# Second gated layer of tiles 0 and 1 with held weights and 512 moving tokens, turned back by VectorE during the next tile

## The chip, the cores and the metric

The program runs on one core of a Trainium2 chip. A core has a matrix engine (TensorE, PE in the profile, with PEld for its weight loads), a vector engine (VectorE, DVE), a scalar engine (ScalarE, ACT), GpSimd (POOL) and a queue engine (SyncE, SP) that issues nearly all DMAs here. Each engine runs its own instructions in order; between engines the order is kept by semaphores. SBUF holds 128 partitions of working memory, PSUM holds what PE writes. The metric is the device time of the whole program in microseconds (us), lower being better.

## The reference

Attention with a decay, then a feed-forward layer with a squared ReLU, then a gated feed-forward layer with an RMS norm in front of it, all in float32:

```python
# 4 batches, 8 heads, 768 tokens, 64 wide; afterwards 3072 tokens of 512 features
state = gamma * state + outer(k[t], v[t]);  y[t] = scale * q[t] @ state
h = maximum(x @ w_in, 0);  x = h * h @ w_out                 # 512 -> 2048 -> 512
rms = sqrt(mean(x * x, axis=-1) + 1e-6);  xn = x / rms * rms_g
g = xn @ w_gate;  silu = g * sigmoid(g);  val = xn @ w_val   # 512 -> 1536, twice
out = silu * val @ w_out                                     # 1536 -> 512
```

## The kernel before, in words

Each float32 matrix product is made of seven products of half the size (a Strassen scheme with 7 instead of 8: `OPERAND`, `ITEMS`), and each operand is split into a high and a low float32r part, so that every small product is three matmuls (`three`, L785 to L789). PSUM holds the accumulators X, Y, Z (two banks of 512 columns each); the seven products k = 0 to 6 go to X, Z, Y, X, Y, Z, Y in that order.

The 3072 tokens are three tiles of 1024 tokens, and a tile has two halves, n = 0 and 1, of 512 tokens. After the attention come two layers, each for t = 0, 1, 2. A layer has front runs and then one back run.

- A **front run** (`front_run` on every engine) is seven products of 12 matmuls with 512 moving columns. The second layer (`front2_run` on DVE) has six front runs q = 0 to 5 a tile. When product 0 is done, ACT copies X into Y (`seed`, L982). Product 2 accumulates into Y and so waits for `seeded`, while `seed` waits for `y_taken` of the run before: DVE's last read of Y in that run (`tail`, L1484 to L1491). Between lie ACT's silu (L1014) and a cast of weights (`high_w`, L915). DVE also adds up four weight sums for the next run (`sum_w`, L1361 to L1369).
- A **back run** (`back_run`) multiplies the hidden layer, which lies feature by token in `hid`, with the output weights. It has 21 groups in the second layer (7 products of G2 = 3 groups) and 28 in the first. For each group ACT casts a high part of a hidden operand (`high_hop`, L975), DVE makes the low part (`low_hop`, L1315) in one of three places, DVE also combines operands for later groups (`combine_hop`), and SP fetches a prepared weight item of 512 KB (`load_items`, L474) into one of four places.

In the back run of the first layer the weights are held in PE (stationary) and 512 tokens move: 12 matmuls of 512 columns a group, and the result lies feature by token. In the second layer it is the other way round (L850 to L855): 128 tokens are held and the 256 columns of the weights move, 24 matmuls a group, and the result lies token by feature as `out` needs it. There the norm's factor `rinv` is one number per partition and is applied while X, Y, Z are read: ACT's `scale_tokens` (L986, four instructions of 256 columns) and DVE's L1608 and L1621. A result (A, Dd, Bb, C are the four quarters: two halves of the tokens by two halves of the features) goes to `out_sb`, which is `hid[:, 6:8]`, and SP stores it with `store_out` within the same back run, the last quarter early in the next tile.

The order on each engine is the order of the code. In a front run SP first waits for the last weight part of the run (`w_lo`), issues the next 1 MB of raw weights (`load_raw_w`, L402), then other loads; in run q = 5 of tiles 0 and 1 it also loads 2 MB for the next tile's front (`load_front`, L510), and then the first four items of the back run.

Of the kernel before, what the change touches and what calls it, by code (L numbers as in the profile page):

```python
# [1 line left out]

# [7 lines left out]
ALU = mybir.AluOpType  # L10
# [109 lines left out]
def build(nc, qkv, decay_mask, decay_q, decay_s, decay_k, w_f1, w_f2, w_b, rms_g, out):  # L120
# [6 lines left out]
    with ExitStack() as ctx:  # L127
# [18 lines left out]
        warm = sb("warm", [P, 1])  # L146
        rinv_t = sb("rinv_t", [P, TILES, 8])
        sums_q = sb("sums_q", [P, 32])
# [49 lines left out]
        z_taken = sem("z_taken")  # L198
        seeded = sem("seeded")
        p5_saved = sem("p5_saved")  # L200
        u2_saved = sem("u2_saved")
# [153 lines left out]
        def stored_chunks():  # L355
            return [(b, c) for b in range(B) for c in range(CH) if not (b < 2 and c < 4)]

        def tokens(ps):
# [29 lines left out]
        def _(sp):  # L388
# [134 lines left out]
            def store_out(t, i):  # L523

                s = (A, Dd, Bb, C)[i]
                m, n = divmod(s, 2)
                if s == A:
                    sp.wait_ge(x_taken, run_b2(t) + 1)
                elif s == C and t == TILES - 1:
                    for tb in range(4):  # L530
                        row = CH * (n + 2 * (tb // 2)) + 4 + tb % 2
                        sp.wait_ge(last_scaled, tb + 1)
                        sp.dma_start(out_v[:, row, m, :], out_sb[:, s, tb, :]).then_inc(out_stored, 16)
                    return
                elif s == C:
                    sp.wait_ge(y_taken, run_b2(t) + 1)
# [4 lines left out]
                if t < 2:  # L541
                    row = CH * (2 * t + n)
                    sp.dma_start(out_v[:, row:row + 4, m, :], out_sb[:, s]).then_inc(out_stored, 16)
                    return
# [11 lines left out]
            def spread_rinv(t):  # L556

                sp.wait_ge(rinv_turned, t + 1)
                by_block = rinv_dram[t].rearrange("(k s i) -> s k i", s=4, i=32)
                for i in range(4):  # L560
                    sp.dma_start(by_block[i], rinv_q[8 * i:8 * i + 8, :]).then_inc(rinv_stored[t], 16)
                for i in range(4):
                    sp.dma_start(rinv_t[32 * i:32 * i + 32, t, :], rinv_r[:, i, :]).then_inc(rinv_t_loaded[t], 16)

# [10 lines left out]
            def front_run(m, bk=None):  # L575
# [51 lines left out]
            for t in range(TILES):  # L627
                bk = BackRun(t, True)
                for q in range(R2):
                    front_run(M1 + R2 * t + q, bk if q == R2 - 1 else None)  # L630
                load_items(bk, 0, 8)
                if t + 1 < TILES:
                    load_rinv_b(t + 1)
                load_items(bk, 8, 17)
                store_out(t, 0)
                load_items(bk, 17, 20)
                store_out(t, 1)
                load_items(bk, 20, 21)
                store_out(t, 2)
            store_out(TILES - 1, 3)  # L640
            sp.wait_ge(out_stored, 16 * (4 * (TILES - 1) + 10))

# [69 lines left out]
        def _(pe):  # L712
# [111 lines left out]
            def back_run(bk):  # L824

                for n in range(bk.groups):
# [46 lines left out]
        def _(act):  # L873
# [109 lines left out]

            def scale_tokens(dst, ps, t, n):
                for tb in range(4):
                    op = nc.scalar.activation(dst[:, tb, :], tokens(ps)[:, tb, :], ACT.Copy,  # L986
                                              scale=rinv_t[:, t, 4 * n + tb:4 * n + tb + 1])
                return op

            def save_p5(run, scaled=None):  # L990
# [3 lines left out]
                if scaled is None:  # L994
                    nc.scalar.copy(p5[:], Z[:]).then_inc(p5_saved, 1)
                else:
                    scale_tokens(tokens(p5), Z, scaled, 1).then_inc(p5_saved, 1)

            def save_u2(run, scaled=None):
# [4 lines left out]
                if scaled is None:  # L1004
                    nc.scalar.copy(u2[:], Y[:]).then_inc(u2_saved, 1)
                else:
                    scale_tokens(tokens(u2), Y, scaled, 1).then_inc(u2_saved, 1)

# [13 lines left out]
            def tail(run):  # L1022
# [19 lines left out]
                elif t == TILES - 1:  # L1042
                    for tb in range(4):
                        if tb % 2 == 0:
                            act.wait_ge(last_done, tb // 2 + 1)
                        nc.scalar.activation(out_sb[:, C, tb, :], tokens(Y)[:, tb, :], ACT.Copy,
                                             scale=rinv_t[:, t, tb:tb + 1]).then_inc(last_scaled, 1)
# [76 lines left out]
            def back_run(bk):  # L1124

                t, ng, run = bk.t, bk.ng, bk.run
                for n in range(bk.groups):
# [10 lines left out]
                    if not bk.second and t and n == 19:  # L1138
                        root(t - 1)
                    if n == 2 * ng and bk.second:  # L1140
                        act.wait_ge(rinv_t_loaded[t], 64)
                    if n == 2 * ng:
                        save_p5(run, t if bk.second else None)
                    if n == 3 * ng:
                        save_u2(run, t if bk.second else None)
                    if bk.next_front < 2 * TILES:
# [3 lines left out]
                    if n == 4 * ng:  # L1150
                        act.wait_ge(*done(run, 3))
                        if bk.second:
# [3 lines left out]
                            else:  # L1156
                                act.wait_ge(out_stored, 64 * t)
                            scale_tokens(out_sb[:, A], X, t, 0).then_inc(x_taken, 1)
                        else:
# [49 lines left out]
        def _(dve):  # L1209
# [326 lines left out]
            def front2_run(run, m, t, q, bk):  # L1536
# [38 lines left out]
                if t == 0 and q == 1:  # L1575
                    mean_square(TILES - 1)
                if bk:
                    low_hop(bk, 1)

            def back_run(bk):  # L1580

                t, ng, run = bk.t, bk.ng, bk.run
                for n in range(bk.groups):
# [13 lines left out]
                    if n == 5 * ng:  # L1597
                        dve.wait_ge(*done(run, 4))
                        dve.wait_ge(p5_saved, run + 1)
                        if bk.second:  # L1600
                            dve.wait_ge(rinv_t_loaded[t], 64)
                            if t == 0:
                                for j in range(4):
                                    dve.wait_ge(kept[j], 16 * len(range(j, 28, 4)))
                            else:
                                dve.wait_ge(out_stored, 64 * t)
                            for tb in range(4):
                                op = nc.vector.scalar_tensor_tensor(  # L1608
                                    out_sb[:, Dd, tb, :], tokens(Y)[:, tb, :], rinv_t[:, t, 4 + tb:5 + tb],
                                    tokens(p5)[:, tb, :], ALU.mult, ALU.add)  # L1610
                            op.then_inc(c22_done, 1)
# [4 lines left out]
                    if n == 6 * ng:  # L1616
                        dve.wait_ge(*done(run, 5))
                        dve.wait_ge(u2_saved, run + 1)
                        if bk.second:
                            for tb in range(4):  # L1620
                                op = nc.vector.scalar_tensor_tensor(  # L1621
                                    out_sb[:, Bb, tb, :], tokens(Z)[:, tb, :], rinv_t[:, t, 4 + tb:5 + tb],
                                    tokens(u2)[:, tb, :], ALU.mult, ALU.add)
                            op.then_inc(z_taken, 1)
# [90 lines left out]
```

## Time and profile before

| | before |
|---|---|
| time, median of 3 runs | 1083.81 us (1083.79 to 1085.39) |
| profiled execution | 1083.72 us |
| its span, first to last instruction | 1081.9 us |
| PE busy | 1071.8 us (99%) |
| DVE busy | 870.9 us (80%) |
| ACT busy | 606.0 us (56%) |
| POOL busy | 335.2 us (31%) |
| granted TensorE clock | 1.000 of full speed |

The span is taken inside the profiled execution, which lasts 1.82 us longer than it. "Busy" of PE counts overlapping matmuls with modelled ends, so how fast matmuls really follow each other is read from their start times. In a row of a timeline the first number is the start in us, the second the duration; "idle before" is time the engine had nothing to do, with what ended it. Starts of successive instructions on DVE lie closer than their durations, since an instruction's end overlaps the next one's begin.

### The profile page before, as it was taken

How to read it: one execution, taken by the hardware profiler on the slowest of the kernel's cores; microseconds unless marked ns; L12 is line 12 of the kernel's file. 1: busy time of each engine (PE TensorE's matmuls, PEld its weight loads, DVE VectorE, ACT ScalarE, POOL GpSimd, SP SyncE). 2: the span in 40 equal slices, each digit the busy share in tenths (PEclk: the TensorE clock that was granted, in tenths of full speed). 3: DMA queues.
4: the chain of work that ended last, by engine and by line, in shares of the span. 5: the costliest groups of instructions: out<-in, count | busy, mean ns of one | idle time of the engine just before them, and what ended most of it. 6: DMA issues, size and time to landing. Idle time of an engine off the chain costs nothing.

```text
span 1081.9 us, 16730 instructions
## 1 busy us (share of the span) xinstructions
PE 1071.8 (99%) x6492; PEld 920.7 (85%) x6492; DVE 870.9 (80%) x926; ACT 606.0 (56%) x926; POOL 335.2 (31%) x240
## 2 busy tenths in 40 slices
PE   8999999999999999999999999999999999999998
PEld 7888788888888888888888888998888998888898
DVE  4686999878979879889899988878675976867684
ACT  5886565466644666554664545646454555544453
POOL 1764552004450005430034653005444002544000
PEclk9999999999999999999999999999999999999999
DMA  9999548763447644465642336553114563120355
GB/s 355 381 405 410 214 180 284 235 215 117 175 156 238 216 150 163 149 236 197 224 148 92 122 113 234 195 176 99 39 62 161 199 204 116 40 77 1 117 185 185
DMA packets 68301, 196.49 MB, mean 182 GB/s; under 512 B 7680, under 2 KB 22016, under 8 KB 63360
## 3 DMA queue, kind: packets, MB, share of 16 engines
q1 hardware_dynamic: 65776, 191.22, 50.2%
q10 hardware_dynamic: 2448, 4.22, 1.0%
q8 instruction: 52, 0.85, 0.3%
q14 instruction: 25, 0.20, 0.1%
HBM read 152.87 MB, written 42.48 MB: 181 GB/s over the span
## 4 chain that ended last, share of the span: by engine, by line
PE 92%; DMA 3%; ACT 2%; DVE 1%; issue 1%; POOL 1%; ACTq 0%; SPq 0%; DVEq 0%; POOLq 0%
PE Y L787 13%; PE Y L788 13%; PE Y L789 13%; PE Z L787 8%; PE X L787 8%; PE X L788 8%; PE X L789 8%; PE Z L788 8%; PE Z L789 8%; DMA item_scratch<-ops 2%; PE Z L746 1%; PE Z L736 1%; ACT k_dec L903 1%; PE R L763 1%; DMA kv_sb<-qkv 1%
## 5 line engine op out<-in xcount | busy, mean ns | idle before, releaser
L648 POOL TENSOR_TENSOR w_ops<-raw_w,w_ops 128x512 fp32r<-128x512 f32 x90 | 127.6, 1418 | 500.6 <-ACT w_ops L915 500.5
L975 ACT CAST ops<-hid 128x1024 fp32r<-128x1024 f32 x147 | 154.1, 1048 | 162.6 <-PE Z L789 55.8
L1315 DVE TENSOR_TENSOR ops<-hid,ops 128x1024 fp32r<-128x1024 f32 x147 | 179.5, 1221 | 50.1 <-ACT ops L975 49.4
L648 POOL TENSOR_TENSOR w_ops<-sums_w,w_ops 128x512 fp32r<-128x512 f32 x120 | 172.8, 1442 | 128.5 <-ACT w_ops L915 128.0
L787 PE MATMUL Y<-ops,w_ops 128*128 128x512 f32 x360 | 140.3, 390 | 1.6 <-DVE hid L1511 1.6
L789 PE MATMUL Y<-ops,w_ops 128*128 128x512 f32 x360 | 140.1, 389 | 0.0
L788 PE MATMUL Y<-ops,w_ops 128*128 128x512 f32 x360 | 140.1, 389 | 0.0
L787 PE MATMUL Y<-ops 128*128 128x256 f32 (+1 forms) x360 | 117.1, 325 | 0.0
L788 PE MATMUL Y<-ops 128*128 128x256 f32 (+1 forms) x360 | 117.1, 325 | 0.0
L789 PE MATMUL Y<-ops 128*128 128x256 f32 (+1 forms) x360 | 117.1, 325 | 0.0
L1014 ACT ACTIVATE gt<-gt 128x512 f32<-128x512 f32 x72 | 45.1, 633 | 118.4 <-DVE gt L1574 41.0
L915 ACT CAST w_ops<-sums_w 128x512 fp32r<-128x512 f32 x120 | 74.3, 621 | 45.2 <-PE Y L789 17.3
L787 PE MATMUL X<-ops,w_ops 128*128 128x512 f32 x240 | 93.4, 389 | 0.0
L788 PE MATMUL X<-ops,w_ops 128*128 128x512 f32 x240 | 93.4, 389 | 0.0
L789 PE MATMUL Z<-ops,w_ops 128*128 128x512 f32 x240 | 93.4, 389 | 0.0
L787 PE MATMUL Z<-ops,w_ops 128*128 128x512 f32 x240 | 93.4, 389 | 0.0
L788 PE MATMUL Z<-ops,w_ops 128*128 128x512 f32 x240 | 93.4, 389 | 0.0
L789 PE MATMUL X<-ops,w_ops 128*128 128x512 f32 x240 | 93.4, 389 | 0.0
L787 PEld LDWEIGHTS Y<-ops,w_ops 128*128 128x128 f32 x360 | 67.6, 188 | 16.5 <-DVE hid L1511 2.3
L1240 DVE TENSOR_TENSOR ops<-raw,ops 128x1024 fp32r<-128x1024 f32 x39 | 56.2, 1446 | 30.8 <-ACT ops L934 30.6
L789 PEld LDWEIGHTS Y<-ops,w_ops 128*128 128x128 f32 x360 | 67.6, 188 | 14.2
L788 PEld LDWEIGHTS Y<-ops,w_ops 128*128 128x128 f32 x360 | 67.6, 188 | 13.8
(159 smaller groups left out, 2475.4 us busy)
## 6 DMA issues: line engine op xcount, KB each, us to landing
ops<-item_scratch SPq DMA_DIRECT2D x147, 512.0 KB, 4.0
raw_w<-w_f SPq DMA_DIRECT2D x30, 1024.0 KB, 4.9
item_scratch<-hid SPq DMA_DIRECT2D x30, 512.0 KB, 3.1
qk_sb<-qkv SPq DMA_DIRECT2D x24, 512.0 KB, 8.5
kv_sb<-qkv SPq DMA_DIRECT2D x20, 512.0 KB, 8.6
y_scratch<-hid SPq DMA_DIRECT2D x12, 512.0 KB, 5.8
raw<-y_scratch SPq DMA_DIRECT2D x3, 2048.0 KB, 9.1
raw<-w_b SPq DMA_DIRECT2D x5, 1024.0 KB, 5.0
```

Of the source, the lines that this page charges most:

```text
L648: nc.gpsimd.tensor_tensor(w_ops[:, k, 1], front_w_source(m, k), f32(w_ops[:, k, 0]), ALU.subtract).then_inc(w_lo, 1)
L736: nc.tensor.matmul(y_ps[rows, p * P:(p + 1) * P], state[rows, p, :], q_dec[rows, c % 2, p * P:(p + 1) * P], start=(p == 0), stop=False, sk ...
L746: mm = nc.tensor.matmul(y_ps[rows, cols], kv_sb[:, n % KVR, V, h * D:(h + 1) * D], masked[:, c % 2, h % 2, cols], start=(c == 0 and h < 2) ...
L763: mm = nc.tensor.matmul(state_ps[head_rows(h), D * p:D * p + D], k_dec[:, c % 2, cols], kv_sb[:, n % KVR, V, cols], start=(c == 0 and p == ...
L787: nc.tensor.matmul(dst, left_hi, right_hi, start=start, stop=False, skip_group_check=True)
L788: nc.tensor.matmul(dst, left_hi, right_lo, start=False, stop=False, skip_group_check=True)
L789: return nc.tensor.matmul(dst, left_lo, right_hi, start=False, stop=True, skip_group_check=True)
L915: nc.scalar.copy(w_ops[:, k, 0], front_w_source(m, k)).then_inc(w_hi, 1)
L975: nc.scalar.copy(hop_at(n)[:, 0], hid[:, 2 * g:2 * g + 2, OPERAND[k], :]).then_inc(hop_hi, 1)
L1014: nc.scalar.activation(gt[:, i % 2, :], gt[:, i % 2, :], ACT.Silu).then_inc(gate_out, 1)
L1240: nc.vector.tensor_tensor(front_lo_at(k), raw_slot(OPERAND[k]), f32(front_hi_at(k)), ALU.subtract).then_inc(front_lo, 1)
L1315: nc.vector.tensor_tensor(hop[:, 1], hid[:, 2 * g:2 * g + 2, OPERAND[k], :], f32(hop[:, 0]), ALU.subtract).then_inc(hop_lo, 1)
```

## The change

The second layer's back runs of tiles 0 and 1 are made like those of the first layer: weights held, 512 tokens moving, 12 matmuls a group. Only tile 2 keeps the old form (`by_token`). The results of tiles 0 and 1 thus lie feature by token. ACT and DVE now read X, Y, Z of these tiles without the factor, as single instructions of 1024 columns. In the next tile, at the end of each front run q = 1 to 4, DVE executes `turn` on one quarter: two transposes of 32x32 blocks through `hid[:, 5]`, which is free then, and one multiplication with `rinv_turn`, a copy of the norm's factors spread over the partitions. In front runs q = 2 to 5 SP issues that quarter's stores, four DMAs of 128 KB each in place of one of 512 KB; a contiguous piece in `out` is 64 columns (256 B) in place of 256 columns (1 KB). So that the 64 columns of a block of partitions lie together, the columns of the output weights are permuted on the host (`turned_columns`), and tile 2 undoes it while it writes `out_sb` (`by_column`, `in_rows`): its DVE additions become 8 instructions of 128 columns in place of 4 of 256.

```diff
+        self.by_token = second and t == TILES - 1
 ...
+            def store_turned(t, i):
+                m, n = divmod((A, Dd, Bb, C)[i], 2)
+                sp.wait_ge(turn_scaled, 4 * t + i + 1)
+                rows = out[S * (2 * t + n):S * (2 * t + n) + N].rearrange("(b j) d -> j b d", j=32)
+                for a in range(4):
+                    place = out_sb[32 * a:32 * a + 32, (A, Dd, Bb, C)[i]].rearrange("j t d -> j (t d)")
+                    cols = slice(2 * P * m + 64 * a, 2 * P * m + 64 * a + 64)
+                    sp.dma_start(rows[:, :, cols], place.rearrange("j (b d) -> j b d", d=64)).then_inc(out_stored, 16)
 ...
                     load_raw_w(m + 2)
-                if m in (M1 + R2, M1 + 2 * R2):
-                    store_out((m - M1) // R2 - 1, 3)
+                if m >= M1 + R2 and (m - M1) % R2 in (2, 3, 4, 5):
+                    store_turned((m - M1) // R2 - 1, (m - M1) % R2 - 2)
 ...
                 load_items(bk, 8, 17)
-                store_out(t, 0)
+                if bk.by_token:
+                    store_out(t, 0)
 ...
                     for q in range(2):
                         first = k < 2 and g == 0 and q == 0
-                        if not bk.second:
+                        if not bk.by_token:
                             for j in range(2):
                                 cols = slice(j * P, j * P + P)
                                 mm = three(dst[:, j, :], slot[:, 0, q, cols], slot[:, 1, q, cols],
 ...
-                    scale_tokens(out_sb[:, C], Y, t, 0).then_inc(y_taken, 1)
+                    nc.scalar.copy(out_sb[:, C].rearrange("p t d -> p (t d)"),
+                                   Y[:].rearrange("p z n -> p (z n)")).then_inc(y_taken, 1)
 ...
                 if t == 0 and q == 1:
                     mean_square(TILES - 1)
+                if t and 1 <= q <= 4:
+                    turn(t - 1, q - 1)
                 if bk:
                     low_hop(bk, 1)
+
+            def turn(t, i):
+
+                s = (A, Dd, Bb, C)[i]
+                flat, place = hid[:, 5, 0:2, :], out_sb[:, s].rearrange("p t d -> p (t d)")
+                turned_rows = flat.rearrange("p z n -> p (z n)").rearrange("p (b f i) -> p b f i", b=16, f=2)
 ...
+                for f in range(2):
+                    op = nc.vector.transpose(turned_rows[:, :, f, :], place[:, N * f:N * f + N])
+                op.then_inc(turned, 1)
+                dve.wait_ge(turned, 4 * t + i + 1)
+                n = s % 2
+                by_block = rinv_turn[:, t, :, 4 * n:4 * n + 4].rearrange("p s k -> p k s").unsqueeze(3)
+                nc.vector.tensor_tensor(place.rearrange("p (k s d) -> p k s d", k=4, s=4),
+                                        flat.rearrange("p z n -> p (z n)").rearrange("p (k s d) -> p k s d", k=4, s=4),
+                                        by_block.to_broadcast([P, 4, 4, 64]), ALU.mult).then_inc(turn_scaled, 1)
 ...
+    def turned_columns(a):
+        return np.asarray(a).reshape(-1, 2, 4, 2, 32).transpose(0, 1, 3, 2, 4).reshape(-1, DM)
```

On PE the first group of a back run of the second layer, tile 0, is shown as it stands in each kernel, with the wait that begins it (L787 is the first matmul of `three`, L809 the same line in the changed file). Before:

```order
L787 MATMUL X<-ops 128x256 [waits item_loaded3,hop_lo,x_taken]
L788 MATMUL X<-ops 128x256
L789 MATMUL X<-ops 128x256
L787 MATMUL X<-ops 128x256
L788 MATMUL X<-ops 128x256
```

and now:

```order
L809 MATMUL X<-ops 128x512 [waits item_loaded3,hop_lo,x_taken]
L810 MATMUL X<-ops 128x512
L811 MATMUL X<-ops 128x512
L809 MATMUL X<-ops 128x512
L810 MATMUL X<-ops 128x512
```

The waits are the same; 24 rows of 256 columns have become 12 of 512.

On DVE this is the end of front run q = 1 of tile 1 and the begin of the next run. Before (L1574 multiplies the gate with the norm, L1484 to L1491 are `tail`, whose last instruction gives `y_taken`, L1361 is the first weight sum):

```order
L1571 TENSOR_TENSOR hid<-Z,u 128x512 [waits x_taken,u2_saved,product_done]
L1572 TENSOR_TENSOR gt<-Z,u 128x512
L1574 TENSOR_TENSOR gt<-gt,rinv_b 128x512 [waits z_taken]
L1484 TENSOR_TENSOR gt<-Y,rinv_b 128x512 [waits h_d,product_done]
L1486 TENSOR_TENSOR hid<-hid,gt 128x512 [waits gate_out]
L1491 TENSOR_TENSOR hid<-gt,Y 128x512 [waits gate_out]
L1361 TENSOR_TENSOR sums_w<-raw_w 128x512 [waits w_lo,raw_w_loaded1]
```

and now, in the changed file's line numbers:

```order
L1602 TENSOR_TENSOR hid<-Z,u 128x512 [waits x_taken,u2_saved,product_done]
L1603 TENSOR_TENSOR gt<-Z,u 128x512
L1605 TENSOR_TENSOR gt<-gt,rinv_b 128x512 [waits z_taken]
L1624 STREAM_TRANSPOSE hid<-hid 128x16x32 [waits rinv_t_loaded0,x_taken]
L1624 STREAM_TRANSPOSE hid<-hid 128x16x32
L1629 TENSOR_TENSOR hid<-hid,rinv_turn 128x1024 [waits turned]
L1515 TENSOR_TENSOR gt<-Y,rinv_b 128x512 [waits h_d,product_done]
L1517 TENSOR_TENSOR hid<-hid,gt 128x512 [waits gate_out]
L1522 TENSOR_TENSOR hid<-gt,Y 128x512 [waits gate_out]
L1392 TENSOR_TENSOR sums_w<-raw_w 128x512 [waits w_lo,raw_w_loaded1]
```

The three instructions of `turn` stand ahead of `tail`, so that `y_taken` comes after them.

On SP this is the end of the last front runs of tile 1. Now, with L413 the raw weights, L563 `store_turned`, L521 `load_front` and L485 the items:

```order
L413 DMA raw_w<-w_f 128x2048 [waits w_lo]
L563 DMA out<-hid 32x16x64 [waits turn_scaled]
L563 DMA out<-hid 32x16x64 x3
L521 DMA raw<-y_scratch 128x4096 [waits y_stored1,y_stored2,y_stored0,y_stored3,quad_lo,front_lo]
L485 DMA ops<-item_scratch 128x1024 [waits product_done] x4
```

Before, the load of `raw` stood directly behind that of `raw_w`.

## Rows read from the trace of the kernel before

**Rows 1.** Chain of waits, shares of the span by engine.

```profile
PE 92%; DMA 3%; ACT 2%; DVE 1%; issue 1%; POOL 1%; ACTq 0%; SPq 0%; DVEq 0%; POOLq 0%
```

**Rows 2.** PE timeline, second layer's back run, tile 0: start, duration, line.

```profile
675.82 0.28 PE L789 MATMUL X<-ops 128*128 128x256 f32 x1
676.51 0.36 PE L787 MATMUL Z<-ops 128*128 128x256 f32 x1 [0.41 <-issue]
676.70 0.28 PE L788 MATMUL Z<-ops 128*128 128x256 f32 x1
676.82 0.28 PE L789 MATMUL Z<-ops 128*128 128x256 f32 x1
...
728.30 0.28 PE L789 MATMUL Y<-ops 128*128 128x256 f32 x1
```

**Rows 3.** PE timeline, first layer's back run, tile 2.

```profile
487.68 0.39 PE L787 MATMUL Z<-ops 128*128 128x512 f32 x1
...
499.92 0.39 PE L787 MATMUL Y<-ops 128*128 128x512 f32 x1
```

**Rows 4.** PE timeline, front run q = 3, tile 1.

```profile
790.78 0.39 PE L789 MATMUL Z<-ops,w_ops 128*128 128x512 f32 x1
791.00 0.39 PE L787 MATMUL Y<-ops,w_ops 128*128 128x512 f32 x1
```

**Rows 5.** DVE timeline, end of front run q = 2, tile 1, and next.

```profile
785.49 0.69 DVE L1574 TENSOR_TENSOR gt<-gt,rinv_b 128x512 f32<-128x512 f32 x1
786.10 0.68 DVE L1484 TENSOR_TENSOR gt<-Y,rinv_b 128x512 f32<-128x512 f32 x1
786.88 0.69 DVE L1486 TENSOR_TENSOR hid<-hid,gt 128x512 f32<-128x512 f32 x1
787.49 0.68 DVE L1491 TENSOR_TENSOR hid<-gt,Y 128x512 f32<-128x512 f32 x1
...
796.64 0.69 DVE L1530 TENSOR_TENSOR gt<-X,rinv_b 128x512 f32<-128x512 f32 x1 [3.75 <-PE X L789]
```

**Rows 6.** ACT timeline, same place.

```profile
786.21 1.24 ACT L1014 ACTIVATE gt<-gt 128x512 f32<-128x512 f32 x2 [2.17 <-DVE gt L1574]
787.35 0.60 ACT L915 CAST w_ops<-raw_w 128x512 fp32r<-128x512 f32 x1
788.48 1.00 ACT L982 COPY Y<-X 128x1024 f32<-128x1024 f32 x1 [0.53 <-PE X L789]
```

**Rows 7.** DVE groups by form: 1024-column multiply, transposes, broadcast multiply.

```profile
L1315 DVE TENSOR_TENSOR ops<-hid,ops 128x1024 fp32r<-128x1024 f32 x147 | 179.5, 1221 | 50.1 <-ACT ops L975 49.4
...
L1234 DVE TENSOR_TENSOR state<-R,decay_s_sb 128x256 f32<-128x256 f32 x20 | 8.3, 417 | 0.0
...
L1417 DVE STREAM_TRANSPOSE gt<-rinv_b 128x1024 f32<-128x1024 f32 x2 | 2.5, 1232 | 0.0
...
L1431 DVE STREAM_TRANSPOSE p<-rinv_b 128x512 f32<-128x512 f32 x1 | 0.7, 714 | 0.0
```

**Rows 8.** DVE timeline, low part of group 3, second layer, tile 0.

```profile
675.18 1.23 DVE L1315 TENSOR_TENSOR ops<-hid,ops 128x1024 fp32r<-128x1024 f32 x1
```

**Rows 9.** Busy time by stretch; last three: clock, DMA share, GB/s.

```profile
724.00:727.00 3.00, 3.00 (x28) 3.00 (x27) 2.90 (x3) 1.41 (x2) 0.00 (x0) 1.00 0.51 175
830.00:832.00 2.00, 2.00 (x10) 1.68 (x9) 0.93 (x2) 0.82 (x2) 1.11 (x1) 1.00 1.05 442
840.00:842.00 2.00, 2.00 (x10) 1.66 (x9) 2.00 (x3) 1.98 (x3) 0.76 (x1) 1.00 0.87 354
842.00:844.00 2.00, 2.00 (x16) 1.88 (x15) 1.97 (x4) 0.43 (x2) 0.88 (x1) 1.00 0.03 12
```

**Rows 10.** SP timeline, front run q = 5, tile 1.

```profile
827.42 0.33 SPq L402 DMA_DIRECT2D raw_w<-w_f  x1
827.98 0.33 SPq L510 DMA_DIRECT2D raw<-y_scratch  x1
834.72 1.28 SPq L474 DMA_DIRECT2D ops<-item_scratch  x3
```

More of the change, by code:

```diff
@@ L1 @@
 from contextlib import ExitStack
+from itertools import product
 import numpy as np
@@ L199, in build @@
         seeded = sem("seeded")
+        turned = sem("turned")
+        turn_scaled = sem("turn_scaled")
         p5_saved = sem("p5_saved")
@@ L356, in stored_chunks, with by_column, in_rows @@
             return [(b, c) for b in range(B) for c in range(CH) if not (b < 2 and c < 4)]
+        def by_column(rows):
+            return rows.rearrange("p (a f i) -> p f a i", a=4, f=2)
+        def in_rows(rows):
+            return rows.rearrange("p (f a i) -> p f a i", f=2, a=4)
         def tokens(ps):
@@ L993, in save_p5, with save_u2 @@
                     act.wait_ge(folded, 2 * TILES)
-                if scaled is None:
+                if not scaled:
                     nc.scalar.copy(p5[:], Z[:]).then_inc(p5_saved, 1)
                 else:
-                    scale_tokens(tokens(p5), Z, scaled, 1).then_inc(p5_saved, 1)
-            def save_u2(run, scaled=None):
+                    scale_tokens(tokens(p5), Z, 1).then_inc(p5_saved, 1)
+            def save_u2(run, scaled=False):
                 if run == 0:
@@ L1003, in save_u2 @@
                 act.wait_ge(*done(run, 2))
-                if scaled is None:
+                if not scaled:
                     nc.scalar.copy(u2[:], Y[:]).then_inc(u2_saved, 1)
                 else:
-                    scale_tokens(tokens(u2), Y, scaled, 1).then_inc(u2_saved, 1)
+                    scale_tokens(tokens(u2), Y, 1).then_inc(u2_saved, 1)
             def silu(run, i):
@@ L1139, in back_run @@
                         root(t - 1)
-                    if n == 2 * ng and bk.second:
+                    if n == 2 * ng and bk.by_token:
                         act.wait_ge(rinv_t_loaded[t], 64)
                     if n == 2 * ng:
-                        save_p5(run, t if bk.second else None)
+                        save_p5(run, bk.by_token)
                     if n == 3 * ng:
-                        save_u2(run, t if bk.second else None)
+                        save_u2(run, bk.by_token)
                     if bk.next_front < 2 * TILES:
@@ L1156, in back_run @@
                             else:
-                                act.wait_ge(out_stored, 64 * t)
-                            scale_tokens(out_sb[:, A], X, t, 0).then_inc(x_taken, 1)
+                                act.wait_ge(out_stored, 256 * t)
+                            if bk.by_token:
+                                for tb in range(4):
+                                    op = nc.scalar.activation(by_column(out_sb[:, A, tb, :]),
+                                                              in_rows(tokens(X)[:, tb, :]), ACT.Copy,
+                                                              scale=rinv_t[:, tb:tb + 1])
+                                op.then_inc(x_taken, 1)
+                            else:
+                                nc.scalar.copy(out_sb[:, A].rearrange("p t d -> p (t d)"),
+                                               X[:].rearrange("p z n -> p (z n)")).then_inc(x_taken, 1)
                         else:
@@ L1605, in back_run @@
                             else:
[L1606 to L1610, printed above, removed]
+                                dve.wait_ge(out_stored, 256 * t)
+                            if bk.by_token:
+                                for tb, f in product(range(4), range(2)):
+                                    op = nc.vector.scalar_tensor_tensor(
+                                        by_column(out_sb[:, Dd, tb, :])[:, f], in_rows(tokens(Y)[:, tb, :])[:, f],
+                                        rinv_t[:, 4 + tb:5 + tb], in_rows(tokens(p5)[:, tb, :])[:, f],
+                                        ALU.mult, ALU.add)
+                            else:
+                                op = nc.vector.tensor_tensor(out_sb[:, Dd].rearrange("p (z t) d -> p z (t d)", z=2),
+                                                             Y[:], p5[:], ALU.add)
                             op.then_inc(c22_done, 1)
@@ L1619, in back_run @@
                         if bk.second:
[L1620 to L1623, printed above, removed]
+                            if bk.by_token:
+                                for tb, f in product(range(4), range(2)):
+                                    op = nc.vector.scalar_tensor_tensor(
+                                        by_column(out_sb[:, Bb, tb, :])[:, f], in_rows(tokens(Z)[:, tb, :])[:, f],
+                                        rinv_t[:, 4 + tb:5 + tb], in_rows(tokens(u2)[:, tb, :])[:, f],
+                                        ALU.mult, ALU.add)
+                            else:
+                                op = nc.vector.tensor_tensor(out_sb[:, Bb].rearrange("p (z t) d -> p z (t d)", z=2),
+                                                             Z[:], u2[:], ALU.add)
                             op.then_inc(z_taken, 1)
```

43 lines of the change are left out of this document (25 added, 18 removed).

## Prediction

> **What bounds the kernel now.** I read the page's table of busy times first (PE is busy 99% of the span), then the chain of waits: 92% of it is PE [rows 1]. So the time is PE's own pace, and two questions decide: how fast PE's instructions follow each other in either form, and whether anything new makes PE wait. The first is read from start times in PE's timeline. In the second layer's back run 432 matmuls of 256 columns start between 676.51 and 728.30, which is 51.79 / 431 = 0.120 us each, so 2.88 us for a group of 24 [rows 2]. In the first layer's back run, with weights held and 512 tokens moving, 54 matmuls lie between two starts, 12.24 / 54 = 0.227 us each, so 2.72 us for a group of 12 [rows 3]. The granted clock is 1.00 (2.4 GHz) in every stretch shown [rows 9]. For the second question I followed the timelines of DVE and ACT over the end of a front run, where the change puts `turn`.
>
> PE hardly waits anywhere. There is one small wait in the stretch concerned: the first matmul of group 3 of tile 0's back run starts at 676.51, where 675.94 would have been its turn [rows 2]. DVE finished the low part of that group's operand at 675.18 + 1.23 = 676.41 [rows 8]. So it is a wait for DVE, though the row calls it "issue", and a wait for a semaphore ends 0.10 us behind its giver. The restart also costs 0.07: the second matmul follows after 0.19 in place of 0.12 [rows 2].
>
> **The change part by part.**
>
> PE in the back runs: 2.88 - 2.72 = 0.16 us less a group, for 2 x 21 groups 6.7 us. But the first three groups of each back run give nothing: group 3 waits for DVE already, DVE's chain up to there (its `tail` of the last front run, then low parts and combinations) is not shortened, and PE arrives earlier only to wait longer. That leaves 2 x 18 x 0.16 = **-5.8 us**. Later groups have cover: DVE needs 1.23 for a low part and about as much for a combination [rows 7, 8], which is 2.4 of 2.72 us, as in the first layer, whose back run holds the pace of 2.72 with the same instructions.
>
> Of the pace itself the Trainium skill says otherwise. Its page "TensorE: Matmul & The Clock Gate", section "Back-to-back issue gap", gives N / 2.4 + 2.5 ns at the high clock: 109 ns for 256 columns and 216 for 512, so 2.62 and 2.59 us a group. By that rule the edit would give 0.03 us a group, 1.1 us over 36 groups, and the change would lose clearly.
>
> The rows show 120 and 227 ns, so 2 x 120 - 227 = 13 ns that the narrow form pays more for the same columns. I go by them, since both shapes are measured in this kernel.
>
> ACT and DVE in the back runs of tiles 0 and 1: reads in one piece of 1024 columns are shorter than four of 256, but neither is late for PE there. Nothing gained, nothing lost. In tile 2 DVE's additions grow from 4 to 8 instructions, hidden by products of 8 us; ACT's last four reads, which end the program, write pieces of 32 columns in place of 256: same count of elements, 0, at most 0.2 us.
>
> DVE's `turn`: two transposes of 512 columns and a multiplication of 1024. One transpose of 512 lasts 714 ns [rows 7], and a successor starts 0.08 before the end (785.49 + 0.69 against 786.10) [rows 5], so 0.63; the second counts full because the multiplication waits for its semaphore, 0.71 + 0.04; the multiplication lasts 1.22 [rows 7] and holds the next one up for 1.14. The factor that is spread over 64 columns costs nothing extra: DVE's row with such a factor has 417 ns for 256 columns [rows 7], which lies on the line of 691 for 512 and 1221 for 1024 [rows 5, 7]. Sum: D = 0.63 + 0.75 + 1.14 = **2.52 us**.
>
> Where it stands. DVE idles 3.75 us in every such front run before L1530 [rows 5], but that idle time is behind the weight sums, and `turn` stands ahead of `tail`. So L1484 starts at 786.10 + 2.52 = 788.62 and ends at 789.30; ACT's last silu 789.34 to 789.97; L1491, which waits for it, 790.00 to 790.69 (before: 787.49 to 788.17). ACT's weight cast goes between and is done at 790.5. `seed` needs L1491 and starts at 790.73 in place of 788.48; before it waited for PE's product 0, and L1491's end at 788.17 plus 0.04 left 0.27 us to spare [rows 5, 6]. It lasts 1.00 and ends at 791.73. PE wants product 2 at 791.00 [rows 4] and starts 0.10 behind `seed`, at 791.83: 0.83 of waiting and 0.07 of restart, **0.90 us**. In short: D less 0.27 less the 1.42 between the old end of `seed` and product 2, plus 0.07, that is D - 1.62. All that follows in this front run is timed by PE and shifts with it, so the next `turn` meets the same picture. The weight sums end at about 795.5 and are needed by nothing before 797; the idle 3.75 us covers those. There are 4 turns in each of tiles 1 and 2: 8 x 0.90 = **+7.2 us**. POOL gets its operands from ACT and has nothing to do while `turn` executes. `turn`'s own waits, for the quarter and for the norm's factors, are over before the front run begins, since both are done in the back run before or earlier.
>
> Bounds of D: with each transpose at 0.61, the pace of a 512-column multiplication [rows 5], and no gap, D = 2.36, 0.74 a turn, +5.9. If blocks of 32 written with a stride cost each transpose the time of the 1024-column row, 1232 ns [rows 7], D = 1.15 + 1.27 + 1.14 = 3.56, 1.94 a turn, +15.5. I take 2.52, since the transposes here move one element a cycle like everything around them.
>
> SP and the stores: 32 DMAs in place of 8, each issued behind `raw_w` in its front run. In runs q = 2 to 4, and in all of tile 2, nothing urgent is queued behind. In q = 5 of tile 1 the 2 MB for the next front and the four items of the back run are. Before, SP issued `raw_w` at 827.42 and `raw` at 827.98, the items from 834.72 on [rows 10], and the engines were empty again by 842 [rows 9]; PE needs item 0 at 842.7. Now `raw_w` comes 2.5 us later (its wait is for POOL's part of `high_w`), the four stores take SP until about 832.5, and `raw` follows. Work for the DMA engines up to item 0: 1 + 2 MB at 442 GB/s [rows 9], 7.1 us; item 0, 1.2; and the stores. 512 KB in pieces of 1 KB occupied the engines for 3 x 0.51 = 1.5 us [rows 9]. Four times as many pieces cost between 1.5 and 6.1; I take 3. From 831.2 on that is 11.3 us, 842.5, against 843.6 that PE's shifted schedule allows, and another 1.1 us would be swallowed by the wait at group 3. So **0**, with up to 2 us if the small pieces cost four times as much.
>
> The Trainium skill warns here: "DMA: Bandwidth & Descriptors", section "Specifications", says transfers under 512 B fall off line rate because they become read-modify-writes. By a doubling for that the stores would occupy the engines 3 us, which is inside the bounds above, and no row here shows stores of 256 B.
>
> Sum: -5.8 + 7.2 + 0 = +1.4 us on a span of 1081.9, 1083.3; with the 1.82 us around the span, and 0.1 for the median over the profiled execution, about **1085.3 us**.
>
> **The rivals.**
>
> 1. The turns are hidden. For: PE shows no wait in the front runs, and DVE has 3.75 us idle there. Against: that idle time lies behind `y_taken`, and only 0.27 + 1.42 us lie on the path from it to product 2. It would give 1083.8 - 5.8 = 1078.0.
> 2. Strided transposes are slow, on the slower side: the block-wise writing in `turn` doubles each transpose to 1.23 us. For: no row has a transpose with a strided output. Against: additions and reductions with pieces go at the full pace. It makes the kernel slower by more than can be overlooked from D = 2.62 upward, where the turns cost 5.8 + 2.2 us; at D = 3.56 the sum is -5.8 + 15.5, so 1093.5.
> 3. The stores delay the items of tile 2's back run, and DMA work also meets other loads: +2 us, 1087.3.
> 4. Columns alone set the pace, and a group of the second layer costs its 2.88 us in either form: 0 + 7.2, 1091.0. For: both forms move the same 6144 columns a group. Against: the first layer's rows have the same tiles, shapes and places and show 2.72. The Trainium skill's page "TensorE: Matmul & The Clock Gate" stands near this rival with its nearly equal 2.62 and 2.59, and would give 1083.8 - 1.1 + 7.2 = 1089.9.
>
> **How the numbers follow.** The forecast has 0.60, with its own range 1084.0 to 1086.9 (D from 2.38 to 2.70). Rival 1 has 0.09, rival 2 0.10, rival 3 0.12, rival 4 0.03, the rest 0.06 spreads on both sides. What a measurement of this kernel can tell from no change is about 0.2%, 2.2 us: 1081.6 to 1086.0. The forecast lies inside, but 0.7 from its upper end, so a fifth of its chance is slower. Faster: rival 1, 0.09, and a little of the rest, 0.10. Slower: 0.12 of the forecast, all of rivals 2 and 4, most of rival 3, some of the rest: 0.36. Same: 0.54. The range of 8 in 10 goes from 1082.6 (D at its lower bound and all 42 groups gaining, 1083.8 - 6.7 + 5.9 = 1083.0, and some of the restart saved) to 1089.5, and leaves out rival 1 and rival 2 at its full price.
>
> **What would show it.** Right: L809 rows in the back runs of tiles 0 and 1 start 0.68 apart in threes; group 3's wait grows to some 0.9 us with the restart; L1624 rows of about 0.71; `seed` starts right behind L1522, the new line of L1491, and PE shows eight waits of 0.8 us before the first Y matmul of product 2 in runs q = 2 to 5 of tiles 1 and 2, and none elsewhere. Wrong: L1624 rows near 1.2 us (rival 2); no waits at product 2 (rival 1); a wait for an item at the start of tile 1's back run (rival 3); a matmul pace other than 0.227 (rival 4); or ACT, not DVE, as the one that `seed` waits for.

## The result and the profile after

The changed kernel takes 1085.96 us (median of 22 runs, 1085.03 to 1088.48) where before takes 1084.3 (22 runs, 1083.3 to 1086.46). The ratio is 1.0014, 95% interval 1.0007 to 1.0020: about 1.5 us slower, less than the 0.2% that I called the least clear change, and the forecast was 1085.3. A gain of 5.7 us and a loss of 7.3 us stand behind it, and both can be read from the trace of the changed kernel (its profiled execution: 1085.6 us, span 1083.8). Among the runs below, one of experiment 3 lasted 3262.7 us, for no reason that its record shows, and the ratio there leaves it out.

From its page, the busy times and the chain of waits:

```profile
PE 1068.7 (99%) x5988; PEld 893.7 (82%) x5988; DVE 894.9 (83%) x946; ACT 601.7 (56%) x902; POOL 338.9 (31%) x240
PE 83%; DVE 6%; ACT 4%; DMA 3%; issue 2%; POOL 1%; ACTq 0%; SPq 0%; DVEq 0%; POOLq 0%
```

Against [rows 1] PE's share of the chain has gone from 92% to 83%, mostly to DVE and ACT. Who waited for whom on PE:

```profile
PE Y L809 <- ACT Y L1004: 4.9, 8, 0.6
PE X L809 <- DMA ops<-item_scratch: 0.6, 1, 0.6
PE Z L809 <- issue: 0.6, 1, 0.6
```

Columns: us in total, times, longest. Eight waits for `seed` (L1004 now), one per turn, none of which was there before; one wait for an item, of which more below; and one wait at group 3 of tile 0's back run.

**The turn, at the place of [rows 5].** DVE's timeline of the changed kernel, end of front run q = 2 of tile 1:

```profile
783.66 0.69 DVE L1605 TENSOR_TENSOR gt<-gt,rinv_b 128x512 f32<-128x512 f32 x1
784.27 1.30 DVE L1624 STREAM_TRANSPOSE hid<-hid 128x512 f32<-128x512 f32 x2
785.60 1.23 DVE L1629 TENSOR_TENSOR hid<-hid,rinv_turn 128x1024 f32<-128x1024 f32 x1
786.74 0.68 DVE L1515 TENSOR_TENSOR gt<-Y,rinv_b 128x512 f32<-128x512 f32 x1
787.34 0.68 DVE L1517 TENSOR_TENSOR hid<-hid,gt 128x512 f32<-128x512 f32 x1
788.13 0.69 DVE L1522 TENSOR_TENSOR hid<-gt,Y 128x512 f32<-128x512 f32 x1
```

The first transpose starts at 784.27 and L1515, which used to start there, at 786.74: D = 2.47 us. ACT at the same place, as [rows 6]:

```profile
784.39 0.63 ACT L1036 ACTIVATE gt<-gt 128x512 f32<-128x512 f32 x1 [2.17 <-DVE gt L1605]
787.46 0.64 ACT L1036 ACTIVATE gt<-gt 128x512 f32<-128x512 f32 x1 [2.44 <-DVE gt L1515]
...
788.90 1.00 ACT L1004 COPY Y<-X 128x1024 f32<-128x1024 f32 x1 [0.30 <-DVE hid L1522]
```

The last silu waits 2.44 us for L1515, and `seed`, which waited for PE before, now waits for DVE's L1522. PE, as [rows 4]:

```profile
788.95 0.39 PE L811 MATMUL Z<-ops,w_ops 128*128 128x512 f32 x1
789.95 0.50 PE L809 MATMUL Y<-ops,w_ops 128*128 128x512 f32 x1 [0.62 <-ACT Y L1004]
790.29 0.40 PE L810 MATMUL Y<-ops,w_ops 128*128 128x512 f32 x1
```

Product 2 was due 0.227 behind the start at 788.95 and starts 0.77 late, 0.05 behind the end of `seed`; the next matmul follows after 0.34, another 0.11. The idle time of 0.62 that the row gives is less than the delay, since it counts from the modelled end of a pipelined matmul. The whole is best read from two equal places of successive runs. At the end of q = 1, before and now:

```profile
766.44 0.69 DVE L1574 TENSOR_TENSOR gt<-gt,rinv_b 128x512 f32<-128x512 f32 x1
```

```profile
763.70 0.69 DVE L1605 TENSOR_TENSOR gt<-gt,rinv_b 128x512 f32<-128x512 f32 x1
```

L1605 starts at 763.70 in q = 1, 783.66 in q = 2, 803.63 in q = 3 and 823.59 in q = 4, so a front run with a turn lasts 19.96 us. Before, the same stretch lasted from 766.44 to 785.49 [rows 5], 19.05. A turn costs 0.91 us.

**The back runs.** The first matmul of tile 0's back run, before and now:

```profile
667.31 0.28 PE L787 MATMUL X<-ops 128*128 128x256 f32 x1
```

```profile
667.42 0.39 PE L809 MATMUL X<-ops 128*128 128x512 f32 x1
```

PE now around group 3 of tile 0's back run, as [rows 2], and at groups 0 and 3 of tile 1's:

```profile
675.68 0.39 PE L811 MATMUL X<-ops 128*128 128x512 f32 x1
676.63 0.47 PE L809 MATMUL Z<-ops 128*128 128x512 f32 x1 [0.56 <-issue]
...
678.09 0.39 PE L809 MATMUL Z<-ops 128*128 128x512 f32 x1
...
678.77 0.39 PE L809 MATMUL Z<-ops 128*128 128x512 f32 x1
...
844.39 0.47 PE L809 MATMUL X<-ops 128*128 128x512 f32 x1 [0.59 <-DMA ops<-item_scratch]
...
852.85 0.47 PE L809 MATMUL Z<-ops 128*128 128x512 f32 x1
```

Three matmuls take 0.68 us, the pace of [rows 3]. Group 3 of tile 0 starts at 676.63, 9.21 us behind the start of the back run, against 676.51 and 9.20 before; so the first three groups gained nothing. The idle time of 0.41 that the row of group 3 gave in [rows 2] is 0.56 now. By start times the delay has grown more, from 0.57 to 0.72 us: the matmul before starts at 675.68, so 675.91 would have been group 3's turn. The rest of what PE was early is spent at group 2, which starts 0.19 late and costs a restart of 0.10. At the first turn (L1605 at 763.70, against 766.44) the kernel is ahead by 2.74; with the 0.12 behind at group 3 that is 2.86 us for 18 groups, 0.159 each.

Tile 1's back run begins late, because item 0 lands late: the matmul before it starts at 843.41, so its turn was 843.64, and it starts at 844.39, 0.75 us late (the row's idle time of 0.59 counts from a modelled end). At group 3 that is swallowed: DVE's low part for it, from the changed kernel's DVE timeline,

```profile
851.52 1.23 DVE L1346 TENSOR_TENSOR ops<-hid,ops 128x1024 fp32r<-128x1024 f32 x1
```

ends at 852.75, and the group starts at 852.85, 9.21 behind the 843.64 at which the back run should have begun, as in tile 0. SP and DMA at that place, as [rows 10] and the last of [rows 9]:

```profile
829.92 0.36 SPq L413 DMA_DIRECT2D raw_w<-w_f  x1
830.32 2.81 SPq L563 DMA_DIRECT2D out<-hid  x4
833.36 2.21 SPq L521 DMA_DIRECT2D raw<-y_scratch  x1
835.67 12.05 SPq L485 DMA_DIRECT2D ops<-item_scratch  x5
```

```profile
842.00:844.00 2.00, 1.80 (x8) 1.14 (x7) 1.97 (x5) 1.07 (x2) 1.64 (x1) 1.00 1.01 412
```

`raw` is issued 5.4 us later than before and takes 2.21 us to issue in place of 0.33, and the DMA engines are still full at 842 to 844 (share 1.01), where they were nearly empty before (0.03).

### The profile page after: what moved, and what is told of

Read it like the earlier page. It is cut to its first block, busy times and chain, and to the rows that moved or that the text cites. A ratio compares the mean times of both kernels' runs of the same rounds, so it can differ in the third digit from the quotient of the medians.

```text
span 1083.8 us, 15742 instructions
## 1 busy us (share of the span) xinstructions
PE 1068.7 (99%) x5988; PEld 893.7 (82%) x5988; DVE 894.9 (83%) x946; ACT 601.7 (56%) x902; POOL 338.9 (31%) x240
## 4 chain that ended last, share of the span: by engine, by line
PE 83%; DVE 6%; ACT 4%; DMA 3%; issue 2%; POOL 1%; ACTq 0%; SPq 0%; DVEq 0%; POOLq 0%
PE Y L809 12%; PE Y L811 12%; PE Y L810 12%; PE X L809 8%; PE X L810 8%; PE X L811 8%; PE Z L809 7%; PE Z L810 7%; PE Z L811 7%; DMA item_scratch<-ops 2%; PE Z L768 1%; PE Z L758 1%; ACT k_dec L925 1%; ACT gt L1036 1%; DVE hid L1624 1%
## 5 line engine op out<-in xcount | busy, mean ns | idle before, releaser
L670 POOL TENSOR_TENSOR w_ops<-sums_w,w_ops 128x512 fp32r<-128x512 f32 x120 | 175.4, 1465 | 115.2 <-ACT w_ops L937 114.7
L809 PE MATMUL Y<-ops,w_ops 128*128 128x512 f32 x360 | 141.3, 392 | 6.2 <-ACT Y L1004 4.9
L809 PE MATMUL Y<-ops 128*128 128x512 f32 (+1 forms) x288 | 104.4, 362 | 0.0
L810 PE MATMUL Y<-ops 128*128 128x512 f32 (+1 forms) x288 | 104.4, 362 | 0.0
L811 PE MATMUL Y<-ops 128*128 128x512 f32 (+1 forms) x288 | 104.4, 362 | 0.0
L809 PE MATMUL X<-ops,w_ops 128*128 128x512 f32 x240 | 93.4, 389 | 0.0
L809 PE MATMUL Z<-ops,w_ops 128*128 128x512 f32 x240 | 93.4, 389 | 0.0
L809 PEld LDWEIGHTS Y<-ops,w_ops 128*128 128x128 f32 x360 | 67.5, 188 | 24.4 <-ACT Y L1004 8.3
L811 PEld LDWEIGHTS Y<-ops,w_ops 128*128 128x128 f32 x360 | 67.6, 188 | 14.3
```

What stands on the lines that cost most here:

```text
L670: nc.gpsimd.tensor_tensor(w_ops[:, k, 1], front_w_source(m, k), f32(w_ops[:, k, 0]), ALU.subtract).then_inc(w_lo, 1)
L809: nc.tensor.matmul(dst, left_hi, right_hi, start=start, stop=False, skip_group_check=True)
L810: nc.tensor.matmul(dst, left_hi, right_lo, start=False, stop=False, skip_group_check=True)
L811: return nc.tensor.matmul(dst, left_lo, right_hi, start=False, stop=True, skip_group_check=True)
```

## The experiments

All ratios are to the kernel before, which ran beside them on the same chip (11 runs of it, 1083.91 us, for the first four; 23 runs, 1084.79 us, for the others).

### 1. The turns moved into the idle time of DVE

```diff
+                if t and 2 <= q <= 5:
+                    turn(t - 1, q - 2)
                 gate_x(run, m)
 ...
-                if t and 1 <= q <= 4:
-                    turn(t - 1, q - 1)
```

Each quarter's stores follow one front run later, the last behind the first eight items of the back run.

> Each turn is moved from the end of front runs q = 1 to 4 to the place behind the weight sums and before L1530's wait in q = 2 to 5, where DVE idles; its stores follow one run later. Theory (a turn costs only because it stands ahead of y_taken): the eight waits at product 2 vanish, POOL may lengthen a turn but 3.75 us of idle time cover it, so 5.8 us below before, about 1078.5, ratio 0.9947. Rival (DVE time as such costs, or transposes disturb PE wherever they stand): like the changed kernel, 1086, ratio 1.0014.

Measured: 1079.3 us, ratio 0.9955 (0.9943 to 0.9967), so 4.9 us (3.6 to 6.2) faster than before, and faster than the changed kernel by some 6 us. The waits for `seed` are gone. Its DVE timeline:

```profile
772.73 0.69 DVE L1402 TENSOR_TENSOR sums_w<-raw_w,sums_w 128x512 f32<-128x512 f32 x1
773.34 1.30 DVE L1626 STREAM_TRANSPOSE hid<-hid 128x512 f32<-128x512 f32 x2
774.67 1.22 DVE L1631 TENSOR_TENSOR hid<-hid,rinv_turn 128x1024 f32<-128x1024 f32 x1
777.17 0.69 DVE L1563 TENSOR_TENSOR gt<-X,rinv_b 128x512 f32<-128x512 f32 x1 [1.27 <-PE X L813]
```

The same three instructions, the same durations, and DVE still idles 1.27 us before it is needed. So the work costs nothing where DVE idles; its place did.

### 2. The turns alone, in the kernel before

```diff
+                if t and 1 <= q <= 4:
+                    spend(t - 1, q - 1)
```

`spend` is two transposes and a multiplication, as in `turn`.

> The kernel before with only two transposes and a multiplication of the same sizes added at the end of front runs q = 1 to 4 of tiles 1 and 2; their results are used by nothing, stores and back runs are unchanged. Theory: eight waits at product 2, +7.2 us, about 1091.5, ratio 1.0067. Rival (the changed kernel's loss comes from its stores or elsewhere, and turns are hidden): 1084.3, ratio 1.000.

Measured: 1092.68 us, ratio 1.0075 (1.0063 to 1.0087), 8.1 us slower (6.8 to 9.4). PE's waits in its trace:

```profile
PE Y L788 <- ACT Y L983: 4.9, 8, 0.6
```

These are the eight waits of the changed kernel, with no change to back runs or stores. The forecast of 7.2 us lies within the interval, and 8 x 0.91 = 7.3 too. Stores and back runs are those of the kernel before, so the rival, that the loss comes from there, is out.

### 3. The changed kernel without its turns

```diff
-                for f in range(2):
-                    op = nc.vector.transpose(turned_rows[:, :, f, :], place[:, N * f:N * f + N])
 ...
+                nc.vector.tensor_tensor(hid[0:1, 5, 0, 0:1], rows, rows, ALU.mult).then_inc(turn_scaled, 1)
```

> The changed kernel without the turns: one tiny instruction gives the semaphore, so the results of tiles 0 and 1 are stored unturned and unscaled by the same 32 small-piece DMAs. Theory: the gain of the back runs alone, 36 groups by 0.16 us, 1084.3 - 5.8 = 1078.5, ratio 0.9947. Rival (all 42 groups gain): 1077.6, ratio 0.9938. Rival (the wide form brings nothing): 1084.3.

Measured: 1079.09 us, ratio 0.9948 (0.9936 to 0.9961), 5.6 us faster (4.2 to 6.9). That is the gain of the back runs by itself. 5.8 and 6.7 both lie in the interval, so the time doesn't tell 36 groups from 42; the trace does, by the start of group 3.

### 4. Only the transposes

```diff
-                by_block = rinv_turn[:, t, :, 4 * n:4 * n + 4].rearrange("p s k -> p k s").unsqueeze(3)
-                nc.vector.tensor_tensor(place.rearrange("p (k s d) -> p k s d", k=4, s=4),
 ...
+                op.then_inc(turn_scaled, 1)
```

> The changed kernel with the transposes of a turn but without its multiplication (results unscaled). The DVE chain ahead of y_taken grows by 1.3 us in place of 2.5, less than the 1.69 us of slack. Theory (cost of a turn = D - 1.62, nothing below 1.69): no waits at product 2, 1078.5, ratio 0.9947. Rival (the cost is proportional to the DVE time): half of 7.4 us, so 1078.5 + 3.8 = 1082.3, ratio 0.998.

Measured: 1078.95 us, ratio 0.9949 (0.9935 to 0.9962). In its DVE timeline L1515 starts 1.22 us later than without turns:

```profile
766.11 1.30 DVE L1624 STREAM_TRANSPOSE hid<-hid 128x512 f32<-128x512 f32 x2
767.33 0.65 DVE L1515 TENSOR_TENSOR gt<-Y,rinv_b 128x512 f32<-128x512 f32 x1
```

and PE has no wait for `seed`. 1.22 us a turn ahead of `y_taken` cost nothing, 2.47 us cost 0.91. A cost proportional to DVE's time would be 3.6 us here (1082.3, ratio 0.998) and lies outside the interval: there is a slack, and only what exceeds it counts.

This trace also shows how much lateness of the items the wait at group 3 can cover. PE starts tile 1's back run at 843.28, 1.54 behind its turn, and group 3 right in its pace:

```profile
843.28 0.47 PE L809 MATMUL X<-ops 128*128 128x512 f32 x1 [1.39 <-DMA ops<-item_scratch]
...
851.56 0.39 PE L809 MATMUL Z<-ops 128*128 128x512 f32 x1
```

Group 3 starts 9.82 behind the turn of the back run (841.74), in place of 9.21, so 0.9 us is covered and 0.6 us is lost, once.

### 5. Twice the transposes

```diff
+                spare_rows = hid[:, 5, 2:4, :].rearrange("p z n -> p (z n)").rearrange("p (b f i) -> p b f i", b=16, f=2)
+                for f in range(2):
+                    nc.vector.transpose(spare_rows[:, :, f, :], place[:, N * f:N * f + N])
```

> The changed kernel with two more transposes in each turn, whose results are used by nothing: D grows by about 1.25 us. Theory (cost = D - 1.62 once over the slack): each turn costs 1.25 us more, 8 x 1.25 = 10 us over the changed kernel, about 1095.7, and PE's waits at product 2 grow from 0.6 to about 1.9 us. Rival (a part of the longer chain finds cover): clearly less than 10 us.

Measured: 1100.03 us, ratio 1.0142 (1.0129 to 1.0155). That is 13.2 us above the changed kernel's 1086.78 in the same batch: more than the 10 us of the theory, and the rival, which had less, is out as well. PE's waits are as expected:

```profile
PE Y L809 <- ACT Y L1004: 14.4, 8, 1.8
```

The rest is TensorE's clock. PE in this kernel after the first such wait, and the two stretches around it (last three columns: clock, DMA share, GB/s):

```profile
770.97 0.61 PE L809 MATMUL Y<-ops,w_ops 128*128 128x512 f32 x1 [1.81 <-ACT Y L1004]
771.38 0.63 PE L810 MATMUL Y<-ops,w_ops 128*128 128x512 f32 x1
771.81 0.63 PE L811 MATMUL Y<-ops,w_ops 128*128 128x512 f32 x1
```

```profile
772.00:773.00 1.00, 1.00 (x4) 0.80 (x3) 1.00 (x2) 0.89 (x2) 1.00 (x1) 0.50 0.84 106
775.00:776.00 1.00, 1.00 (x6) 0.83 (x5) 0.48 (x1) 0.38 (x1) 0.00 (x0) 1.00 0.94 294
```

The granted clock is 0.50 (1.2 GHz) after a wait of 1.81 us and 1.00 again by 775; meanwhile matmuls follow each other after 0.43 us in place of 0.227. L1605 starts at 763.49, 786.25, 809.04 and 830.18: two front runs of 22.8 us with the drop, one of 21.1 without, though the wait before it was the same 1.8 us. So a drop costs about 1.6 us, and not each wait brings it: there are three in this trace for eight waits (the stretches from 771, 795 and 1020 on), 4.9 us. Without a drop a front run is longer than the changed kernel's by 21.14 - 19.96 = 1.18 us, as DVE's D is (3.66 against 2.47). Eight times 1.18 and three drops make 14.3 us, and item 0, late here too, loses another 0.4 at group 3, read as in experiment 4. The spans of the two profiled executions, 1098.1 and 1083.8, differ by 14.3; the changed kernel's runs with a clock of 1.00 have 1085.5 to 1086.5, and 1100.0 lies 13.5 to 14.5 above them.

### 6. Stores in pieces of 1 KB

```diff
+                row = CH * (2 * t + n)
+                for k in range(4):
+                    sp.dma_start(out_v[:, row + k, m, :], out_sb[:, (A, Dd, Bb, C)[i], k]).then_inc(out_stored, 16)
```

> The changed kernel, but each quarter is stored by four DMAs of 128 KB in pieces of 1 KB, as many DMAs, so the result is stored in the wrong places. Theory: PE's wait of 0.6 us for an item at the start of tile 1's back run goes or shrinks, and the time stays at 1086.0, since group 3 waits for DVE anyway. Rival (small pieces cost on PE's path): 0.6 us or more faster, 1085.3 or less.

Measured: 1086.43 us, ratio 1.0015 (1.0006 to 1.0024), beside the changed kernel's 1.0016. Its trace has no wait for an item; in return there are two waits at group 3 in place of one:

```profile
PE Z L807 <- issue: 1.2, 2, 0.6
```

In this trace tile 1's back run begins 0.13 behind its turn, and group 3 starts 9.20 behind that turn; in the changed kernel these are 0.75 and 9.21. So the 256 B pieces do delay the item, and the delay costs nothing, since PE would wait for DVE three groups later. It is the traces that show this: the two intervals of the time are too wide to tell 0.6 us.

The pieces do it by way of SP. Four stores of 1 KB pieces take 2.34 us to issue at this place and the load of `raw` behind them 0.33, where the changed kernel has 2.81 and 2.21.

### 7. The turns right behind the tail

```diff
                     tail(run - 1)
+                    if t and q >= 2:
+                        turn(t - 1, q - 2)
```

> The changed kernel with each turn right behind the tail of its front run, so behind y_taken but ahead of the next run's weight sums, in place of ahead of the tail. Stores stay where they are. Theory (y_taken is the only thing that matters): no waits at product 2, 1078.5 to 1079.3 as with the turns in the idle time. Rival (weight sums 2.5 us later hold ACT's weight casts and seed or save up): part of the loss stays, 1081 or more.

Measured: 1078.51 us, ratio 0.9943 (0.9932 to 0.9955), 6.2 us faster than before (4.9 to 7.4). Against the changed kernel each turn stands three DVE instructions later and nothing else is different. Its DVE timeline:

```profile
765.56 0.68 DVE L1522 TENSOR_TENSOR hid<-gt,Y 128x512 f32<-128x512 f32 x1
766.16 1.30 DVE L1624 STREAM_TRANSPOSE hid<-hid 128x512 f32<-128x512 f32 x2
767.49 1.23 DVE L1629 TENSOR_TENSOR hid<-hid,rinv_turn 128x1024 f32<-128x1024 f32 x1
768.64 1.78 DVE L1392 TENSOR_TENSOR sums_w<-raw_w 128x512 f32<-128x512 f32 x1
```

The weight sums start 2.5 us later and nobody waits. The rival, a part of the loss staying, put the time at 1081 or more and is out. This and experiment 1 beat both kernels; between these two the intervals overlap.

### 8. The changed kernel again

> The changed kernel itself, beside the others on the same chip: 1.0014 of before, about 1085.6.

Measured: 1086.78 us, ratio 1.0016 (1.0007 to 1.0025). In this batch the runs of the kernel before, too, lie between 1083.3 and 1086.9: those above 1085.5 have a mean granted clock of 0.998, and most below 1085 have 1.00. The profiled execution of this kernel has such a clock, and the drop is in the attention, before anything that was changed:

```profile
70.00:80.00 10.00, 8.21 (x114) 7.10 (x112) 6.13 (x10) 8.07 (x24) 5.66 (x5) 0.83 1.03 415
```

PE waits 1.8 us for a load of q and k until 74.22, just ahead of it. Such a drop adds some 2 us to runs of either kernel. A wait of this length does not always bring it: in the trace of the kernel before, PE waits 2.16 us until 13.70 and the clock stays at 1.00, while behind the same wait in experiment 2 the clock is at 0.50 from about 14.1 to 17.5.

## Why the prediction was right

**The gain of the back runs** was forecast as 18 groups by 0.16 for a tile, 2.88 us; the trace shows 2.86, and the changed kernel without turns is 5.6 us faster where 5.8 was forecast. That the first three groups gain nothing is shown by group 3's start, 9.21 behind that of the back run against 9.20. I had put all of PE's wait there at group 3, some 0.9 us with the restart; it is 0.72 and 0.08 at group 3, and 0.29 at group 2.

**The pace** of 0.227 us came back in the second layer. Rival 4 and the formula of the Trainium skill's page "TensorE: Matmul & The Clock Gate", section "Back-to-back issue gap", would have left at most 1.1 us of gain; the measured 5.6 (4.2 to 6.9) excludes both. The prediction took that formula for a stream of matmuls, and the page gives it for a single one; for a stream of weight loads and matmuls it states 131 ns at 512 columns. No row here bears that out either: [rows 3] have 227 ns, and the measurement decides.

**The turn** was forecast with D = 2.52 and a cost of 0.90; measured are 2.47 and 0.91. The parts differ a little and cancel: both transposes together take 1.33 in place of 1.38, PE follows `seed` after 0.05 in place of 0.10, the restart costs 0.11 in place of 0.07 and the next few matmuls follow after 0.230. Eight waits are there, as forecast, in runs q = 2 to 5 of tiles 1 and 2. Experiments 1 to 5 and 7 show the cause from all sides: turns alone cost it, without turns it is gone, half a turn is free, a longer turn costs its excess, and the same turn behind `y_taken` is free.

**The stores** were forecast to cost 0, with item 0 about on time. It was late, and PE with it by 0.75 us: `raw_w` came at 829.92, 2.5 later as forecast, but issuing four stores of 256 B pieces and the load behind them took SP 5.25 us (830.32 to 835.57) where I had counted 2.5. The cover that I named, the wait at group 3, swallowed the delay; experiment 6 shows both halves. That was near its end: I had put the cover at 1.1 us, and experiment 4 shows 0.9. The schedule that I gave for PE, 843.6, is 842.7 - 2.88 + 4 x 0.90 = 843.4 by my own terms; that the trace has 843.64 is chance.

The price for the engines was right, but not for its reason. Between 810 and 818, `raw_w` and the stores of q = 4 keep them busy for 6.0 us, and `raw_w` alone took 3.1 of them before, so the stores take 2.9, forecast 3. I had doubled the 1.5 us of one store in 1 KB pieces because of the smaller pieces. By the same reading the trace of experiment 6, with four DMAs of 1 KB pieces, has 2.3 us: most of the growth came with the four DMAs, and the smaller pieces added 0.6. These traces show no doubling by the smaller pieces.

**The rivals.** 1, hidden turns, is excluded by the eight waits; but it became true once the turns were moved, at 1078.5 where it gave 1078.0. 2, slow strided transposes: they last 668 to 705 ns, less than the contiguous 714 of [rows 7]. 3, the items: the mechanism is there, without a price in the changed kernel, and with 0.6 us in experiment 4.

**The sum** was +1.4, and the traces give -2 x 2.86 + 8 x 0.91 = +1.6 us; the median moved by 1.7. The spans moved by 1.9, of which 0.11 lies ahead of the second layer's back runs. Tile 2's back run, where I had put the permuted writes at 0, lasts 60.47 us from its first matmul's start to its last one's, against 60.46.

What stays open: whether 36 or 42 groups would gain if DVE's chain ahead of group 3 were shorter wasn't tried. Why three of eight equal waits brought the lower clock is not settled by one trace.

## What to carry to other kernels

Idle time of an engine is cover only for work that stands behind what others are waiting for: trace the added instructions along the engine's order to the next semaphore that someone needs, take the slack there (here 1.69 us), and only the excess costs, each time. DVE had 3.75 us of idle time in every run and the turn needed 2.5, but three instructions too early it took back the whole gain; three instructions later it was free. And a wait of PE that grows can cost more than its length, when the clock falls behind it.

## What the runs showed of the hardware

- A 32x32-block transpose of 128x512 float32 on DVE, written in blocks of 32 with a stride, lasts 668 to 705 ns, as a contiguous one (711 to 714).
- PE waits of 0.6 us, eight times, left the granted clock at 1.00; waits of 1.8 us were followed three times in eight by some 3.4 us at 0.50, which cost 1.6 us each (experiment 5). The Trainium skill's page "TensorE: Matmul & The Clock Gate", section "What's actually happening", names these two levels, and the trace agrees.
- In tile 1, four stores of 128 KB in pieces of 256 B took SP 2.7 to 3.2 us to issue, in pieces of 1 KB 2.3 to 2.7 us (experiment 6), against about 0.4 for one store of 512 KB in pieces of 1 KB. Behind the stores of 256 B pieces the issue of a 2 MB load took 2.21 us, behind the others 0.33.
- The same stores occupied the 16 DMA engines for 2.9 us in pieces of 256 B, for 2.3 us in pieces of 1 KB, and as one DMA of 512 KB for 1.5 us.
